# Unread matrix products ahead of and between the first attention tiles, with the first loads cut smaller and the embeddings scaled by a diagonal

## What is computed

```python
# attention: 4 batches x 8 heads, 576 positions, head size 64
scores = (q @ k.T) / 8
thresh = scores.max(-1) - tau
scores = where(scores >= thresh, scores, -1e9)
attn   = exp(scores - scores.max(-1)); attn /= attn.sum(-1) + 1e-9
x      = attn @ v                       # rows: 2304 tokens x 512 features

# experts: each token goes to the best of 8
xn, en = x / (|x| + 1e-6), emb / (|emb| + 1e-6)
logits = xn @ en.T / tau_moe
e      = argmax(logits);  gate = softmax(logits)[e]
x      = gate * (relu(x @ w1[e]) @ w2[e])          # 512 -> 1024 -> 512

# feed-forward, 512 -> 1536 -> 512
out = (silu(x @ w_gate) * (x @ w_val)) @ w_out
```

## Time and profile before

| | |
|---|---|
| time, median of 3 | 1116.09 us (1115.06 to 1118.72) |
| profiled execution | 1117.84 us |
| its span, first to last instruction | 1116.3 us |
| TensorE busy | 1085.7 us, 97% of the span |
| mean granted clock over the span | 0.995 |

### The profile page before, as it was taken

How to read it: one execution, slowest core, us unless ns; L and a number is a source line. 1 busy time by engine, 2 the same in 40 slices (tenths; PEclk the granted TensorE clock), 3 DMA queues, 4 the chain that set the end, 5 groups by cost and what they waited for, 6 DMA issues and landing times.

```text
span 1116.3 us, 19186 instructions
## 1 busy us (share of the span) xinstructions
PE 1085.7 (97%) x6759; PEld 1006.5 (90%) x6760; DVE 550.4 (49%) x955; ACT 499.8 (45%) x880; POOL 227.7 (20%) x217
## 2 busy tenths in 40 slices
PE   7999999999999899999999899999999999999995
PEld 7999999999999778888888799999999999999994
DVE  5677767767877764555543444322322323223221
ACT  5777777787777743554452442221212212212211
POOL 3543355446532111122211100010100100100101
PEclk9999999999999999999999999999999999999998
DMA  5233243235211466555633322010000100100000
GB/s 199 89 110 123 71 161 114 85 116 205 71 36 65 156 224 209 188 198 196 209 125 118 116 85 68 1 57 1 29 29 1 56 0 0 56 0 1 29 1 28
DMA packets 36698, 101.20 MB, mean 91 GB/s; under 512 B 3016, under 2 KB 5320, under 8 KB 36624
## 3 DMA queue, kind: packets, MB, share of 16 engines
q1 hardware_dynamic: 30416, 78.29, 20.6%
q0 software_dynamic: 5904, 21.26, 5.6%
q10 hardware_dynamic: 304, 0.67, 0.2%
HBM read 85.26 MB, written 14.95 MB: 90 GB/s over the span
## 4 chain that ended last, share of the span: by engine, by line
PE 63%; DVE 1%; issue 1%; POOL 0%; ACT 0%; DVEq 0%
PE hb L1307 13%; PE hp L1252 10%; PE yp L1277 10%; PE hp L1321 9%; PE gp L1307 7%; PE vp L1307 7%; PE xb L1321 4%; PE hb L1270 2%; PE xb L1240 1%; PE yp L1292 1%; POOL out L1227 0%; DVE w_lo L1424 0%; DVE r_row_b L1637 0%; DVE ht_lo L1572 0%; PE gp L1377 0%
## 5 line engine op out<-in xcount | busy, mean ns | idle before, releaser
L375 PE MATMUL o_ps<-v_in,prob_t 128*128 128x74 f32 (+1 forms) x1440 | 183.7, 275 | 0.0
L375 PEld LDWEIGHTS o_ps<-v_in,prob_t 128*128 128x128 f32 x1440 | 176.9, 194 | 0.2 <-ACT prob_t L450 0.2
L572 DVE TENSOR_REDUCE neg_max<-scores 128x1 f32<-128x576 f32 x144 | 109.0, 757 | 92.1 <-PE scores L334 91.8
L450 ACT ACTIVATE prob_t<-scores 128x640 f32<-128x640 f32 x144 | 102.0, 708 | 78.2 <-PE scores L344 77.4
L583 DVE SCALAR_TENSOR_TENSOR expo<-scores,thresh,expo 128x576 f32<-128x576 f32 x144 | 116.4, 808 | 0.0
L443 ACT ACTIVATE expo<-scores,neg_max 128x576 f32<-128x576 f32 x144 | 107.3, 745 | 4.6 <-DVE neg_max L572 4.6
L334 PE MATMUL scores<-kt_hi,qt 128*128 128x288 f32 x320 | 103.9, 341 | 4.1 <-DVE kt_lo L724 3.8
L344 PE MATMUL scores<-ident,expo 128*128 128x128 f32 x720 | 104.5, 277 | 3.1 <-DVE expo L583 3.1
L1227 POOL DMA_INDIRECT out<-stage,out_row x18 | 17.7, 985 | 400.8 <-ACT stage L1483 397.1
L1307 PE MATMUL hb<-f_xt_hi,w_hi 128*128 128x384 f32 x288 | 97.4, 338 | 0.0
L1307 PE MATMUL hb<-f_xt_hi,w_lo 128*128 128x384 f32 x288 | 96.6, 335 | 0.0
(11 more groups left out here) (289 smaller groups left out, 2420.7 us busy)
## 6 DMA issues: line engine op xcount, KB each, us to landing
stage<-in_moe_w SPq DMA_DIRECT2D x18, 1024.0 KB, 5.5
stage_more<-in_moe_w SPq DMA_DIRECT2D x14, 1024.0 KB, 8.1
q_raw<-in_q SPq DMA_DIRECT2D x15, 640.0 KB, 6.6
k_raw<-in_k SPq DMA_DIRECT2D x15, 576.0 KB, 5.0
v_in<-in_v SPq DMA_DIRECT2D x16, 370.0 KB, 3.0
ys<-y_out POOLq DMA_DIRECT2D x21, 256.5 KB, 3.2
vt_in<-in_vt SPq DMA_DIRECT2D x16, 320.0 KB, 2.9
stage<-in_moe_w_val SPq DMA_DIRECT2D x3, 1024.0 KB, 5.2
```

The source lines that it names most:

```text
L375: last = nc.tensor.matmul(dst, prob_t[:, g % 3, 128 * c:128 * (c + 1)], src, start=(c == 0), stop=(c == KEY_CHUNKS - 1))
L450: nc.scalar.activation(prob_t[:, g % 3, :], scores[g % 3][:].rearrange("p a c -> p (a c)")[:, 0:KEY_CHUNKS * 128], ACT.Copy).then_inc(s_pt ...
L572: V.tensor_reduce(neg_max[:, t:t + 1], scores[g % 3][:, :, 0:HALF], mybir.AxisListType.XY, ALU.max, negate=True).then_inc(s_max, 1)
```

## The change

1. Before the first needed product TensorE runs four products of 128x128 by 512 columns on a block of ones that nobody reads, and after the `tau` product nine more. Three more run ahead of `probs_t(0)` and of `probs_t(1)`. VectorE first fills 512 columns of `qt` of pair 1 with ones (`s_filler`), and GpSimd's work on pair 1 waits for the first scores, so that it does not overwrite them early.
2. The first query tile (128 columns) is loaded by its own DMA and rounded on its own; the other 384 columns follow in a second DMA, and their rounding comes after the first keys. Tile 0 waits for its own part alone, tile 1 for the rest.
3. The first 576 keys are converted in two halves of 288, on ScalarE and on VectorE, and each half of the scores of tile 0 waits for its own half.
4. The embeddings are stored twice side by side by the host, so the block is 8 x 1026 instead of 8 x 514. They are not scaled on VectorE and transposed any more; instead they are multiplied on TensorE with an 8x8 diagonal (`factors`), which scales and turns them at once. The small steps on the norms are reordered: three of them and one reciprocal before the keys, the rest after the maximum of tile 0.

```diff
+FILLERS = (4, 9, 3)
@@ SyncE
                 if p == 2:
-                    sp.wait_ge(s_split0, 2)
+                    sp.wait_ge(s_split0, 4)
                     sp.wait_ge(s_half, 2)
@@ TensorE
             def scores_tile(g):
                 p, t = g // TILES, g % TILES
-                if t == 0:
-                    if p == 0:
-                        pe.wait_ge(s_split0, 2)
-                    else:
-                        pe.wait_ge(s_split, 2 * p)
+                if t == 0 and p:
+                    pe.wait_ge(s_split, 2 * p)
+                if g == 1:
+                    pe.wait_ge(s_split0, 4)
...
                 for half in range(2):
+                    if g == 0:
+                        pe.wait_ge(s_split0, half + 2)
...
             def embeddings_t():
-                pe.wait_ge(s_const, 2)
-                pe.wait_ge(s_es, 9)
+                pe.wait_ge(s_es, 7)
                 for n in range(HEADS):
-                    last = nc.tensor.transpose(o_ps[1][:, EXPERTS * n:EXPERTS * (n + 1)],
-                                               emb_x[:, n, :, :].rearrange("e s d -> e (s d)"), ident[0:EXPERTS, 0:EXPERTS])
+                    last = nc.tensor.matmul(o_ps[1][:, EXPERTS * n:EXPERTS * (n + 1)], emb_sb[:, 128 * n:128 * (n + 1)],
+                                            factors[:], start=True, stop=True)
+            def keep_warm(n, dst, src):
+                for _ in range(n):
+                    nc.tensor.matmul(dst, src[:, 0:128], src[:, 0:PSUM_BANK], start=True, stop=True)
+
+            pe.wait_ge(s_filler, 1)
+            keep_warm(FILLERS[0], scores[2][:, 0, :], qt[:, 1, :])
             pe.wait_ge(s_ones, 1)
             pe.wait_ge(s_emb, 16)
...
+            keep_warm(FILLERS[1], scores[2][:, 0, :], qt[:, 1, :])
             for g in range(-2, STEPS + 2):
...
                 if g == -1:
                     embeddings_t()
+                if 0 <= g < 2:
+                    keep_warm(FILLERS[2], o_ps[g % 2][:], qt[:, 0, :])
                 if 0 <= g < STEPS:
                     probs_t(g)
@@ ScalarE
-            act.dma_start(q_raw[:, 0, 0:MAIN], q[0, :, 0:MAIN]).then_inc(s_first_q, 16)
+            act.dma_start(q_raw[:, 0, 0:128], q[0, :, 0:128]).then_inc(s_tile_q, 16)
+            act.dma_start(q_raw[:, 0, 128:MAIN], q[0, :, 128:MAIN]).then_inc(s_first_q, 16)
...
-            nc.scalar.activation(kt_hi[:, 0, 0:SEQ], k_raw[:, 0, 0:SEQ], ACT.Copy, scale=k_scale[:]).then_inc(s_first_hi, 1)
+            for half in range(2):
+                keys = slice(HALF * half, HALF * (half + 1))
+                nc.scalar.activation(kt_hi[:, 0, keys], k_raw[:, 0, keys], ACT.Copy, scale=k_scale[:]).then_inc(s_first_hi, 1)
@@ VectorE
+            V.memset(qt[:, 1, 0:PSUM_BANK].bitcast(F32), 1.0).then_inc(s_filler, 1)
             V.memset(warm[:], 1.0).then_inc(s_warm, 1)
+            V.memset(ones[:], 1.0).then_inc(s_ones, 1)
             V.memset(emb_2[:], 0.0).then_inc(s_zero, 1)
-            V.memset(ones[:], 1.0).then_inc(s_ones, 1)
...
-            dve.wait_ge(s_first_q, 16)
-            V.tensor_copy(qt[:, 0, 0:MAIN], q_raw[:, 0, 0:MAIN]).then_inc(s_first_q_hi, 1)
+            dve.wait_ge(s_tile_q, 16)
+            V.tensor_copy(qt[:, 0, 0:128], q_raw[:, 0, 0:128]).then_inc(s_tile_q_hi, 1)
...
+            V.reciprocal(es[:, 3:4], emb_sb[:, 2 * FEAT:2 * FEAT + 1]).then_inc(s_es, 1)
...
+            V.scalar_tensor_tensor(es[:, 2:3], es[:, 2:3], es[:, 0:1], es[:, 1:2], ALU.mult, ALU.add).then_inc(s_es, 1)
+            for half in range(2):
+                keys = slice(HALF * half, HALF * (half + 1))
+                dve.wait_ge(s_first_hi, half + 1)
+                V.scalar_tensor_tensor(kt_lo[:, 0, keys], k_raw[:, 0, keys], k_scale[:], kt_hi[:, 0, keys].bitcast(F32),
+                                       ALU.mult, ALU.subtract).then_inc(s_split0, 1)
+            dve.wait_ge(s_first_q, 16)
+            V.tensor_copy(qt[:, 0, 128:MAIN], q_raw[:, 0, 128:MAIN]).then_inc(s_first_q_hi, 1)
+            dve.wait_ge(s_first_q_hi, 1)
+            V.tensor_tensor(qt[D:128, 0, 128:MAIN], q_raw[D:128, 0, 128:MAIN], qt[D:128, 0, 128:MAIN].bitcast(F32),
+                            ALU.subtract).then_inc(s_split0, 1)
+            max_tile(0)
             dve.wait_ge(s_es, 4)
...
+            V.reciprocal(es[:, 2:3], es[:, 2:3]).then_inc(s_es, 1)
             dve.wait_ge(s_es, 6)
...
+            dve.wait_ge(s_const, 2)
+            V.tensor_scalar(factors[:], ident[0:EXPERTS, 0:EXPERTS], es[:, 2:3], es[:, 3:4],
+                            ALU.mult, ALU.mult).then_inc(s_es, 1)
-            V.tensor_scalar(emb_x[:], emb_sb[:, 0:FEAT].rearrange("e (h s d) -> e h s d", h=HEADS, s=1)
-                            .broadcast_to([EXPERTS, HEADS, 2, D]), es[:, 2:3], es[:, 3:4], ALU.mult, ALU.mult).then_inc(s_es, 1)
@@ GpSimd
             def split(p):
                 par = p % 2
+                if p == 1:
+                    pool.wait_ge(s_scores, 1)
```

More of the change, by code:

```diff
@@ L186, in attention @@
         o_sb = sb("o_sb", [128, 2, TILES, V_COLS])
-        emb_sb = nc.alloc_sbuf_tensor_at("emb_sb", [EXPERTS, FEAT + 2], F32, offset=weights.start)
-        emb_x = nc.alloc_sbuf_tensor_at("emb_x", [EXPERTS, HEADS, 2, D], F32, offset=weights.start + 4096)
+        emb_sb = nc.alloc_sbuf_tensor_at("emb_sb", [EXPERTS, 2 * FEAT + 2], F32, offset=weights.start)
+        factors = nc.alloc_sbuf_tensor_at("factors", [EXPERTS, EXPERTS], F32, offset=weights.start + 4608)
         emb_2 = sb_hole("emb_2", [128, HEADS, 2 * EXPERTS])
@@ L210, in attention @@
         s_first_hi, s_first_q_hi = sem("s_first_hi"), sem("s_first_q_hi")
+        s_tile_q, s_tile_q_hi = sem("s_tile_q"), sem("s_tile_q_hi")
+        s_filler = sem("s_filler")
         s_half_q, s_half = sem("s_half_q"), sem("s_half")
@@ L412, in embeddings_t @@
             def embeddings_t():
-                pe.wait_ge(s_const, 2)
-                pe.wait_ge(s_es, 9)
+                pe.wait_ge(s_es, 7)
                 for n in range(HEADS):
-                    last = nc.tensor.transpose(o_ps[1][:, EXPERTS * n:EXPERTS * (n + 1)],
-                                               emb_x[:, n, :, :].rearrange("e s d -> e (s d)"), ident[0:EXPERTS, 0:EXPERTS])
+                    last = nc.tensor.matmul(o_ps[1][:, EXPERTS * n:EXPERTS * (n + 1)], emb_sb[:, 128 * n:128 * (n + 1)],
+                                            factors[:], start=True, stop=True)
                 last.then_inc(s_et, 1)
+            def keep_warm(n, dst, src):
[3 more added lines that the diff above has]
+            keep_warm(FILLERS[0], scores[2][:, 0, :], qt[:, 1, :])
             pe.wait_ge(s_ones, 1)
             pe.wait_ge(s_emb, 16)
-            nc.tensor.matmul(o_ps[0][:, 0:1], ones[:], emb_sb[0:1, FEAT + 1:FEAT + 2], start=True, stop=True).then_inc(s_tau, 1)
+            nc.tensor.matmul(o_ps[0][:, 0:1], ones[:], emb_sb[0:1, 2 * FEAT + 1:2 * FEAT + 2],
+                             start=True, stop=True).then_inc(s_tau, 1)
+            keep_warm(FILLERS[1], scores[2][:, 0, :], qt[:, 1, :])
             for g in range(-2, STEPS + 2):
@@ L715, in _ @@
             V.tensor_scalar(tau_abs[:], tau_sb[:], -1.0, tau_sb[:], ALU.mult, ALU.max).then_inc(s_tau_done, 1)
-            dve.wait_ge(s_first_q, 16)
-            V.tensor_copy(qt[:, 0, 0:MAIN], q_raw[:, 0, 0:MAIN]).then_inc(s_first_q_hi, 1)
-            dve.wait_ge(s_first_q_hi, 1)
-            V.tensor_tensor(qt[D:128, 0, 0:MAIN], q_raw[D:128, 0, 0:MAIN], qt[D:128, 0, 0:MAIN].bitcast(F32),
+            dve.wait_ge(s_tile_q, 16)
+            V.tensor_copy(qt[:, 0, 0:128], q_raw[:, 0, 0:128]).then_inc(s_tile_q_hi, 1)
+            dve.wait_ge(s_tile_q_hi, 1)
+            V.tensor_tensor(qt[D:128, 0, 0:128], q_raw[D:128, 0, 0:128], qt[D:128, 0, 0:128].bitcast(F32),
                             ALU.subtract).then_inc(s_split0, 1)
             dve.wait_ge(s_tau_done, 3)
-            dve.wait_ge(s_first_hi, 1)
-            V.scalar_tensor_tensor(kt_lo[:, 0, 0:SEQ], k_raw[:, 0, 0:SEQ], k_scale[:], kt_hi[:, 0, 0:SEQ].bitcast(F32),
-                                   ALU.mult, ALU.subtract).then_inc(s_split0, 1)
+            dve.wait_ge(s_emb, 16)
+            V.reciprocal(es[:, 3:4], emb_sb[:, 2 * FEAT:2 * FEAT + 1]).then_inc(s_es, 1)
             dve.wait_ge(s_root, 1)
@@ L1785, in laid_out @@
     taus = [np.full((EXPERTS, 1), arrays.pop(name).item(), np.float32) for name in ("moe_tau", "tau")]
-    arrays["moe_expert_emb"] = np.concatenate([arrays["moe_expert_emb"]] + taus, axis=1)
+    twice = np.repeat(arrays["moe_expert_emb"].reshape(EXPERTS, HEADS, 1, D), 2, axis=2).reshape(EXPERTS, 2 * FEAT)
+    arrays["moe_expert_emb"] = np.concatenate([twice] + taus, axis=1)
     arrays["k"] = np.ascontiguousarray(features_first(arrays["k"], np).reshape(PAIRS, 128, 2 * SEQ))
```

16 lines of the change are left out of this document (6 added, 10 removed).

## The result

The changed kernel takes 1120.01 us (median of 20 executions, 1117.73 to 1124.74) against 1117.16 us before (20 executions, 1115.06 to 1121.65). The ratio is 1.0027, with a 95% interval from 1.0017 to 1.0038: slower by 0.27%, where 1111.0 was forecast.

The account below looks back on a forecast made before the run. TensorE bounds it, at half rate for its first 19 us of tiles. Gains of 0.9 us to tile 3 and 5.0 to tile 6 make 5.9, giving 1111.9 (profiled) or 1110.2 (median); 1111.0 was taken, range 1107.8 to 1114.6.

Parts of the forecast that it names:

- Fillers raise the clock: TensorE's start: streaming unread columns before and into the first scores brings the full rate between 5 and 8.5 us.
- The step from tile 3 to tile 6: TensorE's scores: 12.25 us before, 7.25 after at full rate with the last three fillers; gain 5.0 us.
- Queries that land late, up to 0.5: Second query load at the start: free only if landed by 6.85; landing later costs up to 0.5 us.
- The embeddings' wait: TensorE after tile 1's scores: waits for three small steps and the diagonal after maximum 0, to 9.35 us.
- Sixteen passes, 1.75 us at full rate, 3.5 at half: Embeddings on TensorE: eight plain float32 products replace 1.02 us of transposes, running from 9.35 to 11.1 us.
- a late or interrupted rise: Rival: clock rises only during or behind the own values, at 14 to 17 us; 1113.3 to 1114.8 us, chance 0.16.
- The rival that ends slower: Clock stays low through the embeddings, so the added TensorE work costs 6.0 us more; 1122 to 1124 us, chance 0.06.
- hidden: Rival: something fixed in time (pair 1's load, GpSimd) makes tile 9 wait till 35; 1116 to 1117 us, chance 0.06.
- The bound of "faster": Whole kernel: 0.3% (3.35 us) below before, at 1112.7 us; said to contain the forecast's upper end and half the late rise.
- The upper end of the gain, 6.4: Whole kernel: the gain of 5.9 us was bounded as 4.4 to 6.4 us.
- the 7 of the first slice: TensorE's first 28 us slice: its 7 tenths were read as some 8 us not busy, 7.46 before the first scores.

Follow-up runs that it names:

- Split load: Kernel before plus all fillers, with the first queries in two loads (128 and 384 columns) and rounded in two parts: 1118.1 us, ratio 1.0005.
- norms behind: Kernel before plus all fillers, with the maximum of tile 0 moved ahead of the last steps on the norms: 1117.3 us, ratio 0.9999.
- diagonal: Kernel before plus all fillers, with the embeddings stored twice and turned by the 8x8 diagonal in sixteen passes: 1116.6 us, ratio 0.9995.
- transposes: Changed kernel with the embeddings scaled on VectorE and turned by eight transposes as before: 1118.3 us, ratio 1.0007.

## Why the prediction was wrong

- **Fillers raise the clock: right.** It was up by 7.7 us in the changed kernel (forecast: 5 to 8.5), and fillers on their own gave 1113.4, a gain of 0.40% (0.23 to 0.56), against a forecast of 1111.0 for everything. The step from tile 3 to tile 6 was nearly right too, 7.5 us (13.53 to 21.04) where 7.25 was said.
- **"Queries that land late, up to 0.5": the first failed step.** The load was taken as free if it landed by 6.85, and the bound was not worked from a row. Tile 1 was forecast for 7.8 and came at 10.10, 2.3 us late. The nearest row was there, in the timeline of the kernel before, where the next load of the same queue kept GpSimd waiting until 8.64:

```profile
8.64 1.32 POOL L812 CAST qt<-q_raw 128x768 fp32r<-128x768 f32 x1 [6.92 <-DMA q_raw<-in_q]
```

  The added load took that place and landed at 8.1 to 9.1 in six profiles. By itself, with the waits it makes, it costs 4.7 us (1118.1 against 1113.4).
- **The embeddings' wait: the second.** The forecast had them wait to 9.35, which by its own numbers leaves some 0.5 to 1.0 us of idle time behind tile 1, and put no price on it but the time itself. The 9.35 was also early: in the changed kernel they begin at 12.28, since the maximum of tile 0, forecast for 7.8, came at 10.07 behind the late rounding. Moving that one line onto the kernel with fillers costs 3.9 us.
- **Sixteen passes, 1.75 us at full rate, 3.5 at half: nearly right in size** (1.95 and 3.58 measured), **wrong in effect.** Against eight transposes the forecast counted 0.7 us more, but that set 1.02 us of transposes at half rate against passes at full rate; at full rate both, it is 1.95 against 0.63. Even those 1.3 us are less than the 3.2 that they cost (1116.6 against 1113.4), and the rest fits the fall over them. The formula of the Trainium skill ("TensorE: Matmul & The Clock Gate", "LDWEIGHTS (loading the stationary operand)") has no term for TensorE's clock and would give an estimated 1.7 us in either case; at half rate the sixteen took 0.22 us each, so there the measurement decides against it.
- **The rival "a late or interrupted rise"** was the nearest in mechanism and had 0.16 of chance. It was priced as if the rise came once: up to 3.8 us of the gain. What happened is a fall after the rise that lasted 20 us, over a stretch in which the change had added work (passes 2.6 us, late fillers 2.6 us at half rate). The rival that ends slower had the half rate over that work, and the point at which it decides: a rise at 21 us wins nothing. The final rise was at 30.6. It got 0.06, because I argued that the full rate had held through L351 in the kernel before. There it held in dense surroundings, with no idle time ahead of it. The measured 1120.0 lies in the range of no rival: hidden ended at 1117, slower began at 1122.
- **The chances were added up wrongly too.** The bound of "faster", 1112.7, lies below the forecast's upper end (1113.0) and below all of the late rise (1113.3 to 1114.8), not above them. The upper end of the gain, 6.4, has no working. And the 7 of the first slice is its busy share; the 8 us that are not busy are the other three tenths.
- **The terms don't add.** Split load 4.7, norms behind 3.9 and diagonal 3.2 us would make 11.7 together. The changed kernel is 6.6 above fillers alone. The parts overlap, since the split load delays the norms as well; and once the clock has fallen a second cause for it should cost only its own work, which is argued and not shown. For the same reasons each part taken out by itself won little (0.1 to 2.9 us).
- **Not tried by itself:** the keys in two halves. It is in every run on the changed kernel, so what it gives or costs stays open.

## What to carry to other kernels

Work that only keeps the clock up is worth what the longest thin stretch behind it leaves: list every wait and every run of narrow passes until the dense loop begins, before pricing the fillers. A small load put ahead of others in a busy queue landed hardly sooner (4.9 to 5.4 us against 5.4 to 6.4 for the whole), and pushed all behind it back by one place (GpSimd's share came at 11.38 instead of 8.64). Test such a change part by part on the kernel before: here one part of four was worth 0.40%, and the others together took all of it and more, while taking one of them out of the whole won back 2.9 us at best and never showed what the fillers are worth.

Of the versions run, the kernel before with the fillers alone beats both, 1113.4 against 1117.7 and 1120.0 us.

## Not expected of the hardware

- The granted clock reads 1.00 from the start until its first recorded change. In the kernel without fillers it says 1.00 over 8 to 32 us while the score products are 0.24 us apart until about 22 us. Before a first fall or rise the spacing of the products is the better witness.
- The clock fell with far less standstill than the 4.01 us of the earlier trace rows: after 1.84 us of idle time in the changed kernel, and over sixteen narrow passes with 0.29 us ahead of them. The fall doesn't always stand at its cause: in norms behind and split load it came 1.7 and 1.6 us after TensorE had gone back to work, among products at the full rate. And the profile of transposes has a wait of 1.41 us without a fall in the start. In the changed kernel the clock also fell at 379 us, behind an idle time of 2.03 us between the attention and the experts that the kernel before has too without a fall.
- A VectorE step on 8x8 numbers took 0.28 us, and 0.55, 0.63 and 0.88 us where GpSimd's rounding of queries ran beside it; the 8x1024 step took 0.80 and, with a subtraction of GpSimd begun before it, 1.50, 1.80 and 1.93 us. Where VectorE's 8x1024 step began before the subtraction (three profiles) it kept its 0.80 and the subtraction took 2.23 to 2.37 us instead of 1.80. So the later of the two was the slower one; no run isolates it, and that they stand in each other's way is argued, not shown.
